# Attention and gated MLP in one kernel: squares to PSUM, weight and x scaling on ScalarE, x sums and low parts on GpSimd, a ring of four raw tiles, attention of the first tile spread over the first stage

## The reference

```
qn = q / (norm(q, axis=1) + 1e-06);  kn likewise        # norms over the 6016 rows
a  = softmax(kn.T @ qn / tau)                           # 256 x 256 for each batch
x  = v @ a                                              # 12032 rows of 256
xn = x / sqrt(mean(x*x) + 1e-06) * rms_g
out = (silu(xn @ w_gate) * (xn @ w_val)) @ w_out        # 256 -> 1536 -> 256
```

## Time and profile before

| what | value |
|---|---|
| time, median of 3 runs | 1376.18 us (1375.25 to 1376.29) |
| time of the profiled execution | 1376.46 us |
| its span, first to last instruction | 1374.6 us |
| mean granted PE clock | 0.981 |
| first matmul of the second stage on `ps_p` | 150.43 us |
| a tile of the second stage (s = 2, 3, 5 to 9) | 102.1 us |
| tiles 0, 1, 4, 10, 11 | 115.2, 105.0, 106.0, 99.4, 81.8 us |

### The profile page before, as it was taken

One profiled execution on the slowest core, in us unless ns is written; L12 is line 12 of the kernel. 1 busy time (PEld: TensorE's weight loads), 2 busy tenths in 40 slices (PEclk: granted clock), 3 DMA queues, 4 the chain that ended last, 5 costly groups with the idle time before them and its releaser, 6 DMA issues.

```text
span 1374.6 us, 16549 instructions
## 1 busy us (share of the span) xinstructions
PE 1266.7 (92%) x5736; PEld 1038.2 (76%) x5736; DVE 1057.3 (77%) x1652; ACT 623.1 (45%) x1186; POOL 743.3 (54%) x529
## 2 busy tenths in 40 slices
PE   8678698899899999999999999999999999999997
PEld 7567486677687787787787787787787787787797
DVE  3787787887877877876877877877877878877864
ACT  4455543444544444444444444444444444444443
POOL 4974534545545645544644645645545545545654
PEclk9889898999999999999999999999999999999999
DMA  8865102012112112111112112112113012011011
GB/s 286 222 219 174 18 16 62 16 32 70 22 32 68 24 32 71 22 31 55 38 31 61 32 32 68 25 32 71 22 31 77 16 31 73 12 31 47 1 32 24
DMA packets 168597, 77.62 MB, mean 56 GB/s; under 512 B 146498, under 2 KB 162370, under 8 KB 168514
## 3 DMA queue, kind: packets, MB, share of 16 engines
...
## 4 chain that ended last, share of the span: by engine, by line
PE 35%; POOL 28%; issue 20%; DVE 14%; ACT 2%; DMA 1%; SPq 0%; DVEq 0%; POOLq 0%; ACTq 0%
POOL hid_lo L410 13%; PE ps_out L461 10%; POOL vs L417 9%; PE ps_p L461 8%; PE ps_r L461 5%; PE ps_q L461 5%; PE ps_x L461 4%; DVE vs L1034 2%; POOL xo_lo L404 2%; DVE gs L1034 2%; DVE io L993 2%; DVE vt_lo L976 2%; PE ps_out L475 1%; DVE sqr_acc L871 1%; DVE vs L1136 1%
## 5 line engine op out<-in xcount | busy, mean ns | idle before, releaser
L410 POOL TENSOR_TENSOR hid_lo<-vs,hid_hi 128x512 fp32r<-128x512 f32 (+1 forms) x288 | 419.7, 1475 | 543.3 <-ACT hid_hi L761 542.7
L761 ACT ACTIVATE hid_hi<-vs 128x512 fp32r<-128x512 f32 (+1 forms) x288 | 173.1, 618 | 261.2 <-POOL vs L417 172.2
L461 PE MATMUL ps_out<-hid_hi,wo_hi 128*128 128x512 f32 (+1 forms) x576 | 223.1, 387 | 1.3 <-POOL hid_lo L410 1.3
L461 PE MATMUL ps_p<-xo_hi,wc_hi 128*128 128x512 f32 (+1 forms) x432 | 175.3, 406 | 52.3 <-DVE gs L1034 39.0
L461 PE MATMUL ps_out<-hid_hi,wo_lo 128*128 128x512 f32 (+1 forms) x576 | 222.6, 386 | 0.0
L461 PE MATMUL ps_out<-hid_lo,wo_hi 128*128 128x512 f32 (+1 forms) x576 | 222.6, 386 | 0.0
L1034 DVE TENSOR_TENSOR gs<-gs,ps_p 128x512 f32<-128x512 f32 (+1 forms) x216 | 144.6, 670 | 99.8 <-PE ps_p L461 91.9
L417 POOL TENSOR_TENSOR vs<-vs,gs 128x512 f32<-128x512 f32 (+1 forms) x144 | 202.2, 1419 | 34.0 <-DVE vs L1034 34.0
L754 ACT ACTIVATE gs<-gs 128x512 f32<-128x512 f32 (+1 forms) x216 | 134.1, 621 | 179.2 <-DVE gs L1034 176.5
L1034 DVE TENSOR_TENSOR vs<-vs,ps_p 128x512 f32<-128x512 f32 (+1 forms) x216 | 145.0, 671 | 42.1 <-PE ps_p L461 26.4
L461 PE MATMUL ps_p<-xo_lo,wc_hi 128*128 128x512 f32 (+1 forms) x432 | 167.8, 389 | 0.0
(11 more groups left out here) (150 smaller groups left out, 2262.9 us busy)
## 6 DMA issues: line engine op xcount, KB each, us to landing
...
```

Of the source, the lines that this page charges most:

```text
L410: nc.gpsimd.tensor_tensor(hid_lo[:, item, 0:w], src[:, 0:w], fl(hid_hi[:, item, 0:w]), ALU.subtract)\
L461: last = nc.tensor.matmul(ps, lhs[a], rhs[c], start=start and i == 0, stop=stop and i == 2, skip_group_check=goes_on)
L761: nc.scalar.activation(hid_hi[:, item, 0:w], src[:, 0:w], ACT.Copy).then_inc(hid_hi_done, 1)
```

## The change

1. `squares` write to PSUM: two tensors of two banks, `ps_rp` and `ps_qx`, hold `ps_r`, `ps_p`, `ps_q`, `ps_x`, and in the first stage the squares. `add_squares` on DVE reads them there. Norms, attention and transposes of tile 0 therefore use two banks of `ps_out` in turn, and the second stage waits for the last `add_squares`.
2. `hid_lo`'s place, free now, is a fourth place of the ring `raw`; w_out pieces get buffers of their own, so that SP issues two of them after group 17 and the third after 21.
3. `scale_piece` (POOL) becomes `piece_scale` (ACT), and `x_scale` moves from DVE to ACT.
4. `vt_low`, `x_mix` and `late_low` move from DVE to POOL for tiles 1 to 11; `x_mix` is now in the order T1, T2, T3, T4.
5. `x_rms` of half 1 is cut in two pieces, batch 1's `inverse_roots` moves from unit 3 to the end of unit 4 of tile 0, `inverse_norms` a phase earlier.
6. v @ a of tile 0 is one piece a group (groups 17 to 20), where it was four pieces in two groups (17, 18).

```diff
-    RING = 3
+    RING = 4
-               over("raw2", [P, 2, GW], "vs", 0)]
-        sqr = over("sqr", [P, 2, GW], "hid_lo", 0)
+               over("raw2", [P, 2, GW], "hid_lo", 0), over("raw3", [P, 2, GW], "vs", 0)]
+        ps_rp = bank("ps_rp", 2)
+        ps_qx = bank("ps_qx", 2)
+        sqr = [ps_rp, ps_qx]
...
             def wo_piece(piece):
-                sp.wait_ge(wpiece, GV_PIECES - 1 if piece == 0 else GV_PIECES)
+                if piece < 2:
+                    sp.wait_ge(norms_mm, 1)
+                else:
+                    sp.wait_ge(wo_done, piece - 1)
...
-                if G == 20:
+                if G == 17:
                     wo_piece(0)
-            wo_piece(1)
-            wo_piece(2)
+                    wo_piece(1)
+                if G == 21:
+                    wo_piece(2)
...
         @block.gpsimd
-            def scale_piece(u):
...
+            def x_mix(s, i):
+                out, a, b, w = mix_operands(s, i)
+                if i == T1:
+                    pool.wait_ge(x_turned, 2 * s + 2)
+                    pool.wait_ge(x_split, 2 * s + 2)
+                else:
+                    pool.wait_ge(x_mixed, 4 * s + i - T1)
+                if i == T2:
+                    pool.wait_ge(late_split, 5 * s)
+                nc.gpsimd.tensor_tensor(out[:, 0:w], a[:, 0:w], b[:, 0:w], ALU.subtract).then_inc(x_mixed, 1)
...
                     if G > 0:
-                        finish(G - 1)
-                    if s + 1 < TILES and u == 4:
+                        hid_low(G - 1, 1, vs[:, 2, :])
+                        if u == 0:
+                            late_low(s, T4)
+                            late_low(s, B22)
+                        hid_low(G - 1, 2, vs[:, 0, :])
+                        hid_low(G - 1, 3, vs[:, 1, :])
+                    if more and u == 0:
+                        vt_low(s + 1, 0)
...
+                    if more and u == 4:
                         x_lo(s + 1, B11)
                         x_lo(s + 1, B21)
+                        x_mix(s + 1, T1)
+                        x_mix(s + 1, T2)
+                    if more and u == 5:
+                        x_mix(s + 1, T3)
+                        x_mix(s + 1, T4)
+                        late_low(s + 1, T2)
+                        late_low(s + 1, T1)
                     hid_low(G, 0, vs[:, 3, :])
                     multiply(G, 1, vs[:, 2, :], gs[:, 2, :], c22_done)
                     multiply(G, 2, vs[:, 0, :], gs[:, 0, :], c21_done)
+                    if more and u == 5:
+                        late_low(s + 1, T3)
...
         @block.scalar
+            def piece_scale(u):
+                act.wait_ge(piece_in[u % 2], 32 * (u // 2 + 1))
+                part = piece_buf[u % 2].rearrange("p (s h f) -> p h s f", s=2, h=H)
+                for h in range(H):
+                    last = nc.scalar.activation(part[:, h, :, :], part[:, h, :, :], ACT.Copy, scale=gcol[:, h:h + 1])
+                last.then_inc(scaled, 1)
...
+            def x_scale(s, half):
+                act.wait_ge(newton, NEWTON * (2 * s + half + 1))
+                for j in range(width(s)):
+                    part = io[:, half, j * C:(j + 1) * C]
+                    last = nc.scalar.activation(part, part, ACT.Copy, scale=rinv[:, half, j:j + 1])
+                last.then_inc(xn_done, 1)
```

More of the change, by code:

```diff
@@ L363, in chain @@
                 pool.wait_ge(pool_seq, seq[0])
-            def scale_piece(u):
-                pool.wait_ge(piece_in[u % 2], 32 * (u // 2 + 1))
-                part = piece_buf[u % 2].rearrange("p (s h f) -> p h s f", s=2, h=H)
-                for h in range(H):
-                    last = nc.gpsimd.tensor_scalar(part[:, h, :, :], part[:, h, :, :], gcol[:, h:h + 1], None,
-                                                   ALU.mult)
-                chain(last)
             def mix_piece(u):
@@ L681, in wo_hi_piece @@
             def wo_hi_piece(piece):
-                act.wait_ge(piece_in[piece], (32 * 4, 32 * 4, 32)[piece])
+                act.wait_ge(wo_in[piece % 2], 32 * (piece // 2 + 1))
                 fs = slice(WO_CHUNKS * piece, WO_CHUNKS * (piece + 1))
                 for h in range(H):
-                    last = nc.scalar.activation(by_block(wo_hi, fs, h), piece_block(piece, h), ACT.Copy)
-                last.then_inc(wpiece_hi, 1)
+                    last = nc.scalar.activation(by_block(wo_hi, fs, h), piece_block(piece % 2, h), ACT.Copy)
+                last.then_inc(wo_hi_done, 1)
             def copy_spread(b, ps):
@@ L837, in _ @@
                         exponentials(1)
+                    if more and u == 0:
+                        vt_high(s + 1, 0)
                     if more and u == 1:
@@ L850, in _ @@
                     hid_high(G, 0, vs[:, 3, :], h11_done, G + 1)
-                    if more and u == 0:
-                        vt_high(s + 1, 0)
+                    if more and u == 2:
+                        x_scale(s + 1, 0)
+                    if more and u == 3:
+                        x_scale(s + 1, 1)
                     if more and u == 5:
@@ L1011, in x_mix @@
+                inv_sqrt(rinv[:, half, 0:n], ssq[:, half, 0:n], n, newton, base + 1, parts)
+            def x_mix(s, i):
+                out, a, b, w = mix_operands(s, i)
+                if i == T1:
+                    dve.wait_ge(x_turned, 2 * s + 2)
                     dve.wait_ge(x_split, 2 * s + 2)
-                    ins = nc.vector.tensor_tensor(b21, b21, t, ALU.subtract)
-                ins.then_inc(x_mixed, 1)
+                else:
+                    dve.wait_ge(x_mixed, 4 * s + i - T1)
+                nc.vector.tensor_tensor(out[:, 0:w], a[:, 0:w], b[:, 0:w], ALU.subtract).then_inc(x_mixed, 1)
@@ L1067, in _ @@
                 for h in range(H):
-                    last = nc.vector.tensor_copy(xf[:, 2 * half + h, :], first_banks[2 * half + h][:, :])
+                    last = nc.vector.tensor_copy(xf[:, 2 * half + h, :], ps_first[h][:, :])
                 last.then_inc(x_turned, 1)
-                add_squares(GROUPS + 9 + half)
-            for k in range(4):
-                x_mix(0, k)
+                add_squares(GROUPS + 10 + half)
+            for i in (T1, T2, T3, T4):
+                x_mix(0, i)
             for i in LATE:
@@ L1117, in _ @@
                         x_rms(s + 1, 0)
+                    if more and u == 3:
+                        x_rms(s + 1, 1, (1,))
                     if more and u == 4:
                         turn_x(s + 1, 1, 1)
+                    if s == 0 and u == 5:
+                        inverse_norms()
                     q = 2 * G + 1
```

283 lines of the change are left out of this document (131 added, 152 removed).

## The result

The changed kernel takes 1281.39 us (median of 4 runs, 1278.68 to 1283.05), where the kernel before takes 1375.93 beside it. The ratio is 0.9312, 95% interval 0.9295 to 0.9328: 6.9% faster. The sign came as forecast and both stages gained, and the forecast gain was too small: 74.8 us, where 95.0 lie between the two profiled executions (1376.46 and 1281.47).

A forecast was written before the change was run, and what follows sets the result against it. It took POOL's scaling and PE's late v @ a to hold the first stage, transfers only at times, and PE nearly to bound the second, idle behind DVE sums; 27.5 + 47.3 = 74.8 us saved, 1301.7 us, range 1284 to 1326.

The forecast's parts named there:

- the term of a tile: Second stage, each of seven like tiles: idle times removed plus faster POOL products less the tile's edge, 4.3 us saved.
- The five idle times, 5.0: Second stage: PE's five idle times behind late DVE sums, 3.8 us plus 0.25 a restart, 5.0 us a tile.
- The rest, 0.6: Second stage: POOL's own products get faster without DVE's two-input work and the snapshot comes earlier, 0.6 us a tile.
- The edge, -1.3: Tile's edge: POOL's added low parts make PE stall twice by 0.5 us, with restarts 1.3 us a tile lost.
- Rival 2: Second stage: stalls move to POOL at the tile's edge, 1.5 us saved a tile, 1332 us, halfway 1317; chance 0.17.
- First stage, 27.5: From start to first `ps_p` matmul: ACT's order decides, `ps_p` starts at 123 us, 27.5 us saved.
- SP's ring waits: First stage, a sign: SP's waits for a ring place fall below 35 us in total.
- Tile 0, 4.5: Second stage, tile 0: batch 1's inverse-root stall of 6.46 us stays unchanged, so the tile saves 4.5 us.
- Tiles 1, 4, 10 and 11: Second stage, tiles that differ: savings of 5.0, 4.0, 3.0 and 0.7 us.
- Scaling on ACT at nothing: Second stage: x's scaling adds some 3.5 us a tile to ACT where it waits for POOL; nothing taken.
- Rival 4: Transfers at their floor and almost no stall at the edge: 96 us saved, 1280 us; chance 0.11.
- rival 5: Slower than before: POOL becomes the bound of units 4, 5 and 0, about 1400 at 2.0 us each; chance 0.02.

The follow-up runs named there:

- late_tiny: The changed kernel with the late low parts of x on GpSimd cut to 4 columns from tile 5 on: 1272.3 us, tile 7 95.62 us.
- scale_dve: The changed kernel with only the second stage's scaling of x (eight instructions a tile) back on DVE: 1295.8 us, tile 3 97.86 us.
- low_dve: The changed kernel with thirteen low parts and x sums a tile back on DVE, x's scaling left on ACT: 1316.4 us, tile 3 100.12 us.
- late_dve: The changed kernel with only the five late low parts of a tile back on DVE: 1287.9 us, tile 3 97.21 us.
- ring3: The changed kernel with three ring places for the pieces of q and k in place of four, squares still in PSUM: 1282.4 us.
- sqr_sbuf: The changed kernel with the squares written to SBUF again and three ring places: 1300.4 us.

## Why the prediction was too cautious

The step that failed is the term of a tile, **5.0 + 0.6 - 1.3 = 4.3 us**: it measures 5.6, and times the seven tiles of one kind that is 39.9 for 30.1, half of the miss. Its parts:

- *The five idle times, 5.0.* Right in sum. Between the kernel before and `late_tiny`, where the edge costs nothing, units 0, 1, 3 and 5 differ by 0.70 + 1.04 + 1.66 + 1.87 = 5.27. The single ones are off: at 0.25 a restart, units 0 and 5 were priced at 1.07 and 1.50.
- *The rest, 0.6.* Too small. Units 2 and 4 give 0.42 + 0.81 = 1.23, and none of the idle rows speaks of them. I looked for stalls in PE's idle times alone. Unit 4 by windows, first of the kernel before, then of the changed one:

```profile
544.00:559.80 15.80, 15.70 (x68) 12.31 (x66) 12.39 (x18) 7.08 (x14) 11.47 (x9) 1.00 0.46 101
```

```profile
490.30:505.30 15.00, 15.00 (x68) 12.42 (x67) 10.22 (x15) 6.99 (x14) 13.18 (x11) 1.00 0.53 106
```

  The same 68 matmuls at full clock take 0.7 us more of busy PE. Most of it is two late starts, of the kernel before; the last row is ACT's:

```profile
544.72 0.39 PE L461 MATMUL ps_r<-xo_hi,wc_lo 128*128 128x512 f32 x1
545.19 0.50 PE L461 MATMUL ps_p<-xo_hi,wc_hi 128*128 128x512 f32 x1
545.52 0.39 PE L461 MATMUL ps_p<-xo_lo,wc_hi 128*128 128x512 f32 x1
...
559.39 0.39 PE L461 MATMUL ps_q<-xo_hi,wc_lo 128*128 128x512 f32 x1
559.84 0.50 PE L461 MATMUL ps_r<-xo_hi,wc_hi 128*128 128x512 f32 x1
```

```profile
559.18 0.60 ACT L749 ACTIVATE gs<-ps_r 128x512 f32<-128x512 f32 x1 [1.07 <-POOL vs L417]
```

  In an unbroken row starts are 0.23 us apart; here they are 0.47 and 0.33, and 0.45. The recorded end of the matmul before covers nearly all of it, and 0.08 and 0.05 us are left as idle time. The one at 559.84 is PE's wait for ACT's snapshot, which had waited for POOL's product: this is the mechanism that the 0.6 was given for. The runs show what it comes with: unit 2's 0.42 with the scaling (`scale_dve`), unit 4's 0.8 with the x sums (it is in `low_dve` and not in `late_dve`).
- *The edge, -1.3.* It costs 0.88 (`late_tiny`). The place and the engine named were right.

The bounds of a tile's term don't come out of their own terms. An edge that costs as much as the first and last idle time with their restarts takes 0.82 + 1.25 + 0.50 = 2.57 us and leaves 3.0 us a tile, not 1.5; with no edge 5.6 are left, not 6.0. Rival 2 and the upper end of the range rest on that 1.5.

The other terms:

- *First stage, 27.5:* 30.4 measured, within the bounds. The price of a sum from PSUM came as said (1.2 us for 1.21), and so did ACT's chain: group 18's squares begin at 79.4 us (81 forecast), the last square ends at 113.8 (116), and `ps_p` starts at 120.6 (123).

```profile
112.97 0.81 ACT L723 ACTIVATE ps_qx<-raw 128x768 f32<-128x768 f32 x1 [0.26 <-DVE sqr_acc L946]
```

```profile
120.61 0.50 PE L507 MATMUL ps_rp<-xo_hi,wc_hi 128*128 128x512 f32 x1 [2.76 <-DVE xo_lo L1082]
```

  SP's ring waits did not: 48.8 us for less than 35, and the fourth place that was to let the transfers run on is worth 0.3 to 3 us (`ring3`). The share of the squares was underrated: the prediction has none of their saving on the path by itself, and `sqr_sbuf` with the ring loses 19 to 22 us.
- *Tile 0, 4.5:* 7.9. The stall of the inverse roots is there as forecast:

```profile
212.32 0.79 PE L507 MATMUL ps_rp<-xo_hi,wc_hi 128*128 128x512 f32 x1 [6.29 <-DVE gs L1098]
```

  with 14 matmuls in 5.7 us at a granted clock of 0.54 behind it, near the lower of the two levels. Missed was a second stall: unit 5 of tile 0 took 18.90 us before, 2.05 more than tile 3's, with an idle 1.67 us behind batch 1's inverse norms, which the change makes a phase earlier. Units 4 and 5 together went from 44.12 to 40.00.
- *Tiles 1, 4, 10 and 11:* 5.7, 5.6, 4.9 and 0.5 for 5.0, 4.0, 3.0 and 0.7. 4 and 10 are in the main the mistake of a tile again.
- *Scaling on ACT at nothing:* right as far as the runs show; no PE idle time in units 2 and 3 is left.

Terms against measure: first stage 2.9 us, seven tiles 9.8, tile 0 3.4, the four others 4.0. That is 20.1 of the 20.2 us of the miss. Rival 4 had the nearest time, 1280, and half of its reason: its "almost no stall at the edge" (5.5 a tile) is the size seen, but the transfers weren't at their floor, so its nearness is in part luck.

That elementwise work costs more on GpSimd, the premise of rival 5, has its number (1.29 us a low part for 0.68 on DVE undisturbed) and doesn't decide: PE waited for DVE's place in the queue, and POOL had 44.2 us of waiting in a tile.

The Trainium skill (SBUF — State Buffer, Who interferes with whom) says that a DVE instruction with two SBUF inputs contends with a GpSimd instruction that reads SBUF. The traces agree: a low part of two SBUF inputs takes 0.684 us with POOL at rest and a sum of two 1.288 beside it, and a Newton step takes 1.18 us with both operands in SBUF and 0.16 with one of them in PSUM. The Trainium skill also says there that `tensor_scalar` can enter modes which take the shared ports, under conditions on its operands; the two steps of 1.08 and 1.20 us with a single SBUF input agree. So the prediction's words, that one with a single SBUF input doesn't contend, are too wide, though they hold for the additions that it used them for.
